# The drain of an attention stage reordered on five engines, and TensorE's flag branch with the token mixers in both arms

## The chip, the cores and the metric

One Trainium2 chip, one of its cores. The metric is the device time in microseconds (us) of one execution of the program. The kernel before takes 621.71 us, the median of 3 runs (621.22 to 622.42).

## The reference

Three layers in float32, one after the other. The input is 4 batches, 8 heads, 768 tokens, 48 features a head.

```python
# 1: gated linear attention, per head, token by token
state = f[t][:, None] * state + outer(k[t], v[t])      # f = sigmoid(f_logit)
y[t]  = q[t] @ state
# 2: token mixer on x = y with the heads side by side (768 x 384 per batch)
theta = x @ w_theta
mix   = w_tok_r @ (x * cos(theta)) + w_tok_i @ (x * sin(theta))
u     = x + mix
x2    = u + relu(u @ w_ch)
# 3: gated net
h = relu(x2 @ w_in);  u, v = halves of h;  v = layernorm(v)
out = (u * (w_spatial @ v + b_spatial)) @ w_out
```

## The kernel before, in words

**Attention** works on 16 pairs of heads, in a software pipeline. `pipeline(eng, stages)` gives each engine a list of (step, lag). In round n, a step with lag L handles pair n - L. Within a round an engine keeps strictly to its list. Rounds 16 to 19 (20 on SyncE) are the drain: no new pair begins and the last one, pair 15, runs out. Its PSUM banks are four `att_ps` (scores), `kt_ps`, `kv_ps` and two `y_ps`. A pair's result leaves as `y_out` (ScalarE, y_ps to y_sb) and `store` (SyncE, y_sb to the DRAM tensor xT). `y_out` of pair p waits until the store of pair p - 2 has landed.

All matmuls of the later layers are split: a float32 operand becomes a high and a low part (`split_hi` on ScalarE, line 73; `split_lo` on VectorE, line 78), and `three` (line 1054) issues hi x hi, hi x lo and lo x hi.

**The token mixer** handles a batch in six blocks s of 128 tokens. For each block: `turn(s)` on TensorE (three transposes into small_ps) and `xn_out(s)` on ScalarE; `theta(s)` on TensorE (9 matmuls into theta_bank); `to_turns(s)` on ScalarE; `reduce(s)` on VectorE (four operations); `trigs(s)` on ScalarE (abs, sin, cos); `multiply(s)` on VectorE; `z_up(s)` on ScalarE and `z_down(s)` on VectorE split the product z. Then `mix(s, third)` on TensorE: three thirds of 12 matmuls each into the six mix_ps banks. For the first batch each block also needs its part of the mixing weights: a load, `weights_up(s)` on ScalarE, `weights_down(s)` on VectorE. TensorE's list is mix(0,0), theta(2), mix(0,1), turn(3), mix(0,2), mix(1,0), theta(3), mix(1,1), turn(4), and so on. theta_bank and small_ps share PSUM with att_ps 0 and 1, mix_ps 0 to 5 with att_ps 2 and 3, kt_ps, kv_ps, y_ps 0 and 1.

The work on block 0 of the first batch is laid into attention's drain. SyncE's `load_first` (round 16, behind `load_rest` of pair 15 and ahead of the store of pair 11) loads w_theta (576 KB), both halves of x (576 KB each) and the weights of blocks 0 and 1 (768 KB each). ScalarE: `theta_hi` (round 17, last but y_out), `first_x` (round 18: x_hi and the Sin table load), `first_angles` (round 19, ahead of y_out of pair 15: weights_up(0), xn_out(0), to_turns(0), trigs(0)), `first_z` behind the pipeline. TensorE: `first_theta` (turn(0), theta(0); round 19, ahead of `attended` of pair 15), then turn(1) and theta(1) behind the pipeline. VectorE: `theta_lo` and `first_x` in round 18, weights_down(0) to z_down(0) behind the pipeline.

**The flag.** The fast attention is valid only for bounded decays. `row_tops` and `turn_tops` find the largest sum, VectorE writes `flag`, and each engine runs a branch of its own on it: with the flag set, the engines redo attention in another form (`attention_any_decay`). Here the flag is 0 and every engine jumps over that body. The mixers' code stands behind it. The remaining weights (blocks 2 to 5 and w_ch) are loaded by SyncE's `rest`, once the last store has landed (`load_weights`, line 1263).

## Time and profile before

| | |
|---|---|
| median of 3 runs | 621.71 us |
| the profiled execution | 619.17 us |
| its span, first to last instruction | 617.2 us |
| mean granted TensorE clock | 0.989 |
| TensorE matmuls busy (PE) | 580.9 us, 94% |
| VectorE (DVE) busy | 367.0 us, 59% |
| ScalarE (ACT) busy | 290.6 us, 47% |
| GpSimd (POOL) busy | 34.7 us, 6% |
| TensorE idle behind "issue" ahead of mix_ps | 2.0 us |
| TensorE idle behind "issue" ahead of gate_ps | 4.1 us |

Attention takes the first 121 us or so, the token mixer runs to about 363 us, the gated net to the end. In the page of 40 slices (15.4 us each) TensorE's digits are 9 but for the first slice (0), the last (8), and the seventh to ninth, from about 93 to 139 us: 8, 7, 8. That is the end of attention and the start of the token mixer. A share of busy time is an average over stages; what a change of the drain is worth is read from the drain's own rows.

### The profile page before, as it was taken

What the parts mean: (1) busy time and instruction counts of PE and PEld (TensorE: products, weight loads), DVE (VectorE), ACT (ScalarE), POOL (GpSimd) and SP (SyncE); (2) the same over time, 40 slices, a digit from 0 to 9 for tenths busy, and PEclk for the clock granted to TensorE, in tenths of its full rate; (3) what the DMA queues carried; (4) which work ended last, traced back from release to release, by engine and by line L of the source; (5) the groups of instructions that cost most, each with busy time, mean ns of one, the idle gap of its engine ahead of it and who ended that gap; (6) DMA issues with size and microseconds to landing.
All of it is one profiled execution on the core that took longest, in us unless ns stands there. A gap on an engine that the chain in (4) does not pass through costs nothing.

```text
span 617.2 us, 11905 instructions
## 1 busy us (share of the span) xinstructions
PE 580.9 (94%) x4226; PEld 559.9 (91%) x4226; DVE 367.0 (59%) x614; ACT 290.6 (47%) x509; POOL 34.7 (6%) x66
## 2 busy tenths in 40 slices
PE   0999998789999999999999999899999999999998
PEld 0888887689999999999999998898999899989997
DVE  7899998466776538454955557557145713571151
ACT  5799996765553335242644225415331533153112
POOL 3232332000000000000000000000000000000000
PEclk9999999879999999999999999899999999999999
DMA  7879999262410231022013243500040001000102
GB/s 187 201 228 246 267 252 314 59 219 93 192 38 27 65 102 39 25 76 89 0 43 115 76 144 109 207 2 1 25 129 2 0 25 51 0 1 27 52 0 78
DMA packets 31546, 58.76 MB, mean 95 GB/s; under 512 B 3728, under 2 KB 23184, under 8 KB 31504
## 3 DMA queue, kind: packets, MB, share of 16 engines
q1 hardware_dynamic: 31504, 58.21, 31.4%
q8 instruction: 25, 0.41, 0.3%
q14 instruction: 17, 0.14, 0.1%
HBM read 44.04 MB, written 14.16 MB: 94 GB/s over the span
## 4 chain that ended last, share of the span: by engine, by line
PE 72%; DVE 3%; issue 3%; ACT 1%; DMA 1%; DVEq 0%; ACTq 0%; SPq 0%
PE mix_ps L1054 24%; PE gate_ps L1054 16%; PE ringc L1054 10%; PE theta_bank L1054 10%; PE small_ps L1054 10%; PE small_ps L1436 1%; DVE stats L1998 1%; DVE w_lo L78 1%; DMA wc_stage<-in_wC_dram 1%; ACT w_hi L73 0%; ACT v L1848 0%; DVE vn L2016 0%; DVE ang L1574 0%; DVE ang L1571 0%; DVE z L1590 0%
## 5 line engine op out<-in xcount | busy, mean ns | idle before, releaser
L1054 PE MATMUL mix_ps<-w_lo,z_hi 128*128 128x384 f32 x288 | 97.3, 338 | 2.0 <-issue 2.0
L1054 PE MATMUL mix_ps<-w_hi,z_hi 128*128 128x384 f32 x288 | 99.0, 344 | 0.0
L1054 PE MATMUL mix_ps<-w_hi,z_lo 128*128 128x384 f32 x288 | 97.6, 339 | 0.0
L1054 PE MATMUL gate_ps<-w_hi 128*128 128x384 f32 x192 | 64.9, 338 | 4.1 <-issue 4.1
L1054 PE MATMUL gate_ps<-w_hi,w_lo 128*128 128x384 f32 x192 | 64.7, 337 | 0.0
L1054 PE MATMUL gate_ps<-w_lo,w_hi 128*128 128x384 f32 x192 | 64.7, 337 | 0.0
L1054 PEld LDWEIGHTS mix_ps<-w_hi,z_lo 128*128 128x128 f32 x288 | 54.6, 190 | 2.2 <-issue 2.2
L1054 PEld LDWEIGHTS mix_ps<-w_lo,z_hi 128*128 128x128 f32 x288 | 54.6, 190 | 0.0
L1054 PEld LDWEIGHTS mix_ps<-w_hi,z_hi 128*128 128x128 f32 x288 | 54.6, 189 | 0.0
L73 ACT ACTIVATE g_hi<-gate 128x384 fp32r<-128x384 f32 x32 | 16.8, 526 | 78.6 <-DVE gate L2048 78.6
L2044 DVE TENSOR_TENSOR gate<-gate_ps,b_all 128x384 f32<-128x384 f32 x32 | 17.8, 557 | 59.7 <-PE gate_ps L1054 59.5
L78 DVE TENSOR_TENSOR xt_lo<-xt,xt_hi 128x1152 fp32r<-128x1152 f32 x16 | 21.4, 1352 | 45.8 <-ACT xt_hi L73 45.8
L1054 PEld LDWEIGHTS gate_ps<-w_hi 128*128 128x128 f32 x192 | 36.6, 191 | 4.3 <-issue 4.3
L1590 DVE TENSOR_TENSOR z<-z,xn 128x384 f32<-128x384 f32 x48 | 24.6, 555 | 26.0 <-ACT z L1321 26.0
L1304 ACT ACTIVATE turns<-theta_bank 128x384 f32<-128x384 f32 x24 | 11.8, 490 | 53.4 <-PE theta_bank L1054 53.4
L1054 PEld LDWEIGHTS gate_ps<-w_lo,w_hi 128*128 128x128 f32 x192 | 36.5, 190 | 0.0
L1054 PEld LDWEIGHTS gate_ps<-w_hi,w_lo 128*128 128x128 f32 x192 | 36.5, 190 | 0.0
L1315 ACT ACTIVATE turns<-ang 128x384 f32<-128x384 f32 x24 | 12.6, 526 | 49.2 <-DVE ang L1578 49.2
L411 PE MATMUL kt_ps<-heads_first,ks 112*128 112x112 f32 x80 | 12.1, 286 | 20.1 <-DVE ks L560 20.0
L468 PE MATMUL y_ps<-att,v_raw 128*48 128x128 f32 x384 | 26.4, 291 | 3.5 <-ACT y_sb L378 3.5
L411 PEld LDWEIGHTS kt_ps<-heads_first,ks 112*128 112x128 f32 x80 | 8.5, 150 | 23.1 <-issue 17.2
L309 POOL TENSOR_SCALAR_AFFINE_SELECT att<-att 128x384 f32<-128x384 f32 x32 | 27.2, 872 | 33.9 <-ACT att L371 33.9
(163 smaller groups left out, 1417.1 us busy)
## 6 DMA issues: line engine op xcount, KB each, us to landing
f_raw<-in_fT_dram SPq DMA_DIRECT2D x32, 144.0 KB, 3.9
k_raw<-in_kT_dram SPq DMA_DIRECT2D x32, 144.0 KB, 3.3
q_raw<-in_qT_dram SPq DMA_DIRECT2D x32, 144.0 KB, 3.8
v_raw<-in_vC_dram SPq DMA_DIRECT2D x16, 288.0 KB, 4.0
xT<-y_sb SPq DMA_DIRECT2D x32, 144.0 KB, 3.7
xt<-xT SPq DMA_DIRECT2D x8, 576.0 KB, 4.0
w_raw<-in_wB_dram SPq DMA_DIRECT2D x6, 768.0 KB, 6.7
u<-xT SPq DMA_DIRECT2D x8, 576.0 KB, 5.0
```

The costliest lines, as they stand in the source:

```text
L73: return act.activation(hi, x, ACT.Copy)
L78: return dve.tensor_tensor(lo, x, hi.bitcast(F32), ALU.subtract)
L309: pool.affine_select(out=group, in_=group, compare_op=ALU.is_ge, fill=0.0, base=0, pattern=[[0, 3], [1, CHUNK]], channel_multiplier=-1).th ...
L411: last = pe.transpose(kt_ps_[:, c * PAIR:c * PAIR + ROWS], ks[b % 2][:, c * CHUNK:(c + 1) * CHUNK], heads_first[:, :])
L468: pe.matmul(y_ps_[half][rows, cols], values(b, hd, c), att[i][:, n * CHUNK:(n + 1) * CHUNK], start=(c % 3 == 0), stop=False)
L1054: done = pe.matmul(out, a, b, start=(first and n == 0), stop=(last and n == len(terms) - 1))
L1304: act.activation(turns[s % 2][:, :], theta_bank[:, 0:DMODEL], ACT.Copy, bias=MAGIC, scale=TURN_INV).then_inc(turns_done.h, 1)
L1315: act.activation(turns[i][:, :], ang[i][:, :], ACT.Abs).then_inc(mag_done.h, 1)
L1436: last = pe.transpose(small_ps[:, k * 128:(k + 1) * 128], xt[:, k * SEQ + s * 128:k * SEQ + (s + 1) * 128], ident[:, :])
L1590: dve.tensor_tensor(z[i][:, cols], z[i][:, cols], part(xn, s * DMODEL, DMODEL), ALU.mult)\
L1998: dve.bn_stats(stats[i][:, :], v[i][:, :]).then_inc(stats_done.h, 1)
L2044: dve.tensor_tensor(cols, gate_ps[g % 4][:, 0:HALF], part(b_all, th * HALF, HALF), ALU.add)\
```

## The change

It changes the order of steps in the drain, where two waits of TensorE stand, and how TensorE's code is laid out. The arithmetic is the same.

SyncE: w_theta is loaded in round 16 ahead of pair 15's own loads; each store now stands ahead of the mixer's loads of its round; x's first half goes in round 16, the weights of block 0 and x's second half in round 17, the weights of block 1 in round 18.

```diff
-            pipeline(sp, [(load_f, 0), (load_rest, 1), (load_first, 1), (store, 5)], 5, 2 * UNROLL)
+            pipeline(sp, [(load_f, 0), (load_theta, 1), (load_rest, 1), (store, 5), (load_first, 1), (load_mixing(0), 2), (load_mixing(1), 3)],
+                     5, 2 * UNROLL)
...
-            def load_early():
-                load(0)(FIRST)
-                load(1)(FIRST)
-                for n in range(2):
-                    sp.dma_start(w_raw[:, weights(n)], wB[:, weights(n)]).then_inc(wb_late[n], 16)
+            def load_first_x():
+                load(0)(FIRST)
+            def load_first_mixing(n):
+                sp.dma_start(w_raw[:, weights(n)], wB[:, weights(n)]).then_inc(wb_late[n], 16)
+                if n == 0:
+                    load(1)(FIRST)
```

ScalarE, TensorE and VectorE, the lists of the pipeline:

```diff
-            pipeline(act, [(neg_logs, 1), (keys_out, 3), (decays, 2), (growths, 2), (scores_copy, 3), (chunk_ends, 2), (theta_hi, 2),
-                           (first_x, 3), (first_angles, 4), (y_out(0), 4), (y_out(1), 4)])
-            m["first_z"]()
+            pipeline(act, [(neg_logs, 1), (keys_out, 3), (theta_hi, 2), (decays, 2), (growths, 2), (scores_copy, 3), (chunk_ends, 2),
+                           (first_turns, 3), (first_z, 4), (y_out(0), 4), (y_out(1), 4), (first_x, 2)])
...
-            pipeline(pe, [(turn, 3), (scores(0), 3), (scores(1), 3), (first_theta, 4), (attended(0), 4), (attended(1), 4), (states, 3),
-                          (carried(0), 4), (carried(1), 4), (turn_tops, 3)])
+            pipeline(pe, [(turn, 3), (scores(0), 3), (scores(1), 3), (attended(0), 4), (attended(1), 4), (turn_tops, 3), (first_theta, 3),
+                          (states, 3), (carried(0), 4), (carried(1), 4)])
...
-            pipeline(dve, [(sums, 2), (scores_out(0), 3), (scores_out(1), 3), (theta_lo, 3), (keep_in_range, 0), (scale_queries, 2),
-                           (scale_keys, 2), (state_sums, 3), (row_tops, 2), (first_x, 3)])
+            pipeline(dve, [(sums, 2), (scores_out(0), 3), (scores_out(1), 3), (first_x, 3), (top_to_flag, 3), (first_angles, 3),
+                           (keep_in_range, 0), (scale_queries, 2), (scale_keys, 2), (state_sums, 3), (row_tops, 2), (theta_lo, 2)])
```

On ScalarE `first_x` is now x_hi(0) alone; `first_turns` is the Sin table load, weights_up(0), xn_out(0), to_turns(0); `first_z` is trigs(0), z_up(0). On VectorE `top_to_flag` is the wait for TensorE's turned tops and the two operations that make the flag (before: behind the pipeline); `first_angles` is weights_down(0), reduce(0); `first_z`, behind the pipeline, is multiply(0), z_down(0).

TensorE's mix: the wait for the low part of z moves from ahead of the block to ahead of the first group's lo x hi products, and both of these products come last in each group. The wait for the y_ps banks moves from ahead of turn(2) to ahead of mix(0,2).

```diff
                     if third == 0:
                         pe.wait_ge(zhi_done.h, zhi_done.at(b, s + 1))
-                        pe.wait_ge(zlo_done.h, zlo_done.at(b, s + 1))
...
+                        for r in range(2):
+                            z = part(z_hi[i], r * DMODEL + d * 128, 128)
+                            pe.matmul(out, z, w_hi[:, weights_of[r]], start=(s == 0 and r == 0), stop=False)
+                            pe.matmul(out, z, w_lo[:, weights_of[r]], start=False, stop=False)
+                        if g == 0:
+                            pe.wait_ge(zlo_done.h, zlo_done.at(b, s + 1))
+                        for r in range(2):
+                            last = pe.matmul(out, part(z_lo[i], r * DMODEL + d * 128, 128), w_hi[:, weights_of[r]],
+                                             start=False, stop=(s == ST - 1 and r == 1))
...
+                def y_banks(b):
+                    if first(b):
+                        for at in y_out:
+                            pe.wait_ge(*at)
                 batches(pe, [
-                    (mix(0, 0), 1), (theta(2), 1), (mix(0, 1), 1), (turn(3), 1), (mix(0, 2), 1),
+                    (mix(0, 0), 1), (theta(2), 1), (mix(0, 1), 1), (turn(3), 1), (y_banks, 1), (mix(0, 2), 1),
```

TensorE's branch: before, `If(flag > 0)` holds the other attention alone and both mixers stand behind it. After, the mixers stand in the arm for flag 0, which comes first, and once more behind the other attention.

```diff
+        @block.tensor
+        def _(pe):
+            def mixers():
+                mixer["tensor"](pe)["rest"]([attended["a_out"]], [attended["y_sbd"]])
+                gated_tensor(pe)
+
+            pe.wait_ge(flag_ready, 1)
+            with pe.If(pe.value_load(flag[0:1, 0:1], min_val=0, max_val=1) < 1):
+                mixers()
+            with pe.Else():
+                any_decay_tensor(pe)
+                mixers()
```

## Rows read from the trace of the kernel before

**Rows 1.** Busy by stretch: the stretch's length; PE, PEld, DVE, ACT, POOL; clock, DMA.

```profile
125.00:130.00 5.00, 3.61 (x12) 3.61 (x12) 2.95 (x6) 3.64 (x6) 0.00 (x0) 0.54 0.66 209
```

**Rows 2.** Timeline, TensorE: start, duration, engine, line, tiles, [idle before <- its releaser].

```profile
101.75 1.34 PE L478 MATMUL y_ps<-qs,state 48*48 48x128 f32 x20
...
108.88 2.80 PE L468 MATMUL y_ps<-att,v_raw 128*48 128x128 f32 x24 [3.48 <-ACT y_sb L378]
...
123.64 0.52 PE L1436 MATMUL small_ps<-ident,xt 128*128 128x128 f32 x3 [2.71 <-ACT xn L1295]
123.93 0.41 PE L1054 MATMUL mix_ps<-w_hi,z_hi 128*128 128x384 f32 x1
126.39 0.48 PE L1054 MATMUL mix_ps<-w_lo,z_hi 128*128 128x384 f32 x1 [2.04 <-issue]
...
145.16 0.34 PE L1054 MATMUL mix_ps<-w_hi,z_hi 128*128 128x384 f32 x1
```

**Rows 3.** The chain that ended last, in order of time: start, length, what.

```profile
126.39 3.68 PE mix_ps L1054 x11
130.06 2.62 PE theta_bank L1054 x9
...
147.40 1.56 PE theta_bank L1054 x9
```

**Rows 4.** Timeline, ScalarE, same columns as rows 2.

```profile
100.34 0.84 ACT L339 ACTIVATE w_dn<-csum 112x768 f32<-112x768 f32 x1 [1.28 <-DVE csum L534]
...
103.08 1.17 ACT L73 ACTIVATE w_hi<-w_raw 128x1152 fp32r<-128x1152 f32 x1
108.24 0.87 ACT L378 ACTIVATE y_sb<-y_ps 112x384 f32<-112x384 f32 x2 [3.99 <-DMA xT<-y_sb]
...
111.40 1.28 ACT L1372 ACT_TABLE_LOAD   x1
...
113.98 1.48 ACT L73 ACTIVATE w_hi<-w_raw 128x1536 fp32r<-128x1536 f32 x1
...
119.23 0.52 ACT L1315 ACTIVATE turns<-ang 128x384 f32<-128x384 f32 x1 [2.54 <-DVE ang L1578]
...
123.00 0.49 ACT L1295 ACTIVATE xn<-small_ps 128x384 f32<-128x384 f32 x1 [0.31 <-issue]
```

**Rows 5.** Timeline, VectorE, same columns.

```profile
105.77 1.35 DVE L78 TENSOR_TENSOR w_lo<-w_raw,w_hi 128x1152 fp32r<-128x1152 f32 x1
...
115.49 1.76 DVE L78 TENSOR_TENSOR w_lo<-w_raw,w_hi 128x1536 fp32r<-128x1536 f32 x1 [0.88 <-ACT w_hi L73]
117.16 0.35 DVE L1565 TENSOR_SCALAR turns<-turns 128x384 f32<-128x384 f32 x1
...
120.78 1.03 DVE L1590 TENSOR_TENSOR z<-z,xn 128x384 f32<-128x384 f32 x2 [1.58 <-ACT z L1321]
122.72 0.96 DVE L78 TENSOR_TENSOR z_lo<-z,z_hi 128x768 fp32r<-128x768 f32 x1 [0.91 <-ACT z_hi L73]
...
133.25 0.36 DVE L1565 TENSOR_SCALAR turns<-turns 128x384 f32<-128x384 f32 x1
...
140.22 0.95 DVE L78 TENSOR_TENSOR z_lo<-z,z_hi 128x768 fp32r<-128x768 f32 x1
```

**Rows 6.** Timeline, SyncE's DMA issues: start, time over which they were issued, line.

```profile
92.20 0.80 SPq L238 DMA_DIRECT2D k_raw<-in_kT_dram  x2
...
97.72 24.52 SPq L265 DMA_DIRECT2D xT<-y_sb  x10
```

**Rows 7.** Timeline of all engines from 119 us, SyncE's issues.

```profile
121.46 0.78 SPq L265 DMA_DIRECT2D xT<-y_sb  x2
...
125.82 1.07 SPq L1263 DMA_DIRECT2D w_raw<-in_wB_dram  x2
```

**Rows 8.** The tile w_raw, its loads of 576 and 768 KB.

```profile
DMA to landing us min/median/max: 4.5/6.2/10.3
```

**Rows 9.** DMA by queue, 124.0 to 124.5 us: packets, MB, share of 16 engines.

```profile
q8 instruction: 1, 0.02, 11.6%
```

More of the change, by code:

```diff
@@ L252, in load_rest, with load_theta, load_mixing, f @@
                              vC[p.times(1), :, :, :].rearrange("h p x -> p h x")).then_inc(v_in[b].h, 16)
+            def load_theta(p, b):
+                if last_pair(p):
+                    sp.dma_start(w_raw[:, W_THETA:W_MIX], wB[:, W_THETA:W_MIX]).then_inc(w_in, 16)
             def load_first(p, b):
                 if last_pair(p):
-                    sp.dma_start(w_raw[:, W_THETA:W_MIX], wB[:, W_THETA:W_MIX]).then_inc(w_in, 16)
                     for c in x_out:
                         sp.wait_ge(c.h, 32 * 3)
-                    m["first"]()
+                    m["first_x"]()
+            def load_mixing(n):
+                def f(p, b):
+                    if last_pair(p):
+                        m["first_mixing"](n)
+                return f
             def store(p, b):
@@ L1039, in _ @@
                 mixer["vector"](dve)["redo"]()
+        return tensor
 def half_of_tokens(t, th, at=0):
@@ L1270, in rest @@
                 sp.wait_ge(mix_done.h, mix_done.at(Step(None, 1, BATCH - 1), GROUPS))
-            return {"open": opened, "first": load_early, "redo": redo, "rest": rest}
+            return {"open": opened, "first_x": load_first_x, "first_mixing": load_first_mixing, "redo": redo, "rest": rest}
         def pool(eng):
@@ L1467, in f @@
                             pe.wait_ge(u_done.h, u_done.at(b.back(1), g + 1))
-                        last = three(pe, mix_ps[g][:, 0:HALF],
-                                     [(both(z_hi[i], z_lo[i], r * DMODEL + d * 128, 128),
-                                       both(w_hi, w_lo, W_MIX + (2 * s + r) * SEQ + th * HALF, HALF))
-                                      for r in range(2)], first=(s == 0), last=(s == ST - 1))
+                        out = mix_ps[g][:, 0:HALF]
+                        at = [W_MIX + (2 * s + r) * SEQ + th * HALF for r in range(2)]
+                        weights_of = [slice(at[r], at[r] + HALF) for r in range(2)]
+                        for r in range(2):
+                            z = part(z_hi[i], r * DMODEL + d * 128, 128)
+                            pe.matmul(out, z, w_hi[:, weights_of[r]], start=(s == 0 and r == 0), stop=False)
+                            pe.matmul(out, z, w_lo[:, weights_of[r]], start=False, stop=False)
+                        if g == 0:
+                            pe.wait_ge(zlo_done.h, zlo_done.at(b, s + 1))
+                        for r in range(2):
+                            last = pe.matmul(out, part(z_lo[i], r * DMODEL + d * 128, 128), w_hi[:, weights_of[r]],
+                                             start=False, stop=(s == ST - 1 and r == 1))
                         if s == ST - 1:
@@ L1530, in redo, with rest @@
                 pe.wait_ge(redone, REDO_ALL)
-            def rest(banks_free):
-                for at in banks_free:
+            def rest(scores_out, y_out):
+                for at in scores_out:
                     pe.wait_ge(*at)
                 turn(2)(FIRST)
+                def y_banks(b):
+                    if first(b):
+                        for at in y_out:
+                            pe.wait_ge(*at)
                 batches(pe, [
-                    (mix(0, 0), 1), (theta(2), 1), (mix(0, 1), 1), (turn(3), 1), (mix(0, 2), 1),
+                    (mix(0, 0), 1), (theta(2), 1), (mix(0, 1), 1), (turn(3), 1), (y_banks, 1), (mix(0, 2), 1),
                     (mix(1, 0), 1), (theta(3), 1), (first_values(0), 2), (first_values(1), 2), (channel(0), 2), (mix(1, 1), 1), (turn(4), 1), (mix(1, 2), 1), (channel(1), 2),
@@ L1907, in _, with tensor @@
                 (y_out, 2), (x_hi, 0), (w_up(5), 1), (gate_up, 1)], 2)
-        @block.tensor
-        def _(pe):
+        def tensor(pe):
             for c in (u_ps, vs_ps, y_ps):
@@ L2129, in attention_and_mixers @@
                              main, tail_hi, tail_lo, qT, kT, fT, vC, xT)
-        attention_any_decay(nc, sems, block, mixer, attended, waits_passed, flag, flag_ready, qT, kT, fT, vC, xT)
+        any_decay_tensor = attention_any_decay(nc, sems, block, mixer, attended, waits_passed, flag, flag_ready, qT, kT, fT, vC, xT)
         @block.sync
@@ L2141, in _ @@
             mixer["scalar"](act)["rest"]([attended["x_out0"], attended["x_out1"]])
-        @block.tensor
-        def _(pe):
-            mixer["tensor"](pe)["rest"]([attended["a_out"], attended["y_sbd"]])
         @block.vector
@@ L2153, in attention_and_mixers @@
                 banks.enter_context(nc.psum_tensor(f"mixer_bank{_}", [128, 512], F32))
-            gated_net(nc, sems, block, gates, mixer, waits_passed, w_hi, w_lo, in_hi, in_lo, xt, xt_hi, xt_lo, eps, early, late, stage,
+            gated_tensor = gated_net(nc, sems, block, gates, mixer, waits_passed, w_hi, w_lo, in_hi, in_lo, xt, xt_hi, xt_lo, eps, early, late, stage,
                       wC, bias, x2T, out)
+        @block.tensor
[9 more added lines that the diff above has]
+                mixers()
 _INS = ["qT", "kT", "fT", "vC", "wB", "wC", "bias"]
```

178 lines of the change are left out of this document (92 added, 86 removed).

## The prediction

> **What bounds the kernel now.** I read the page of slices first, then the timelines of the stretch in which its TensorE digits dip, then the chain of waits. Outside that stretch TensorE issues matmuls back to back almost everywhere, so the end moves only if TensorE's steady work begins earlier. Inside it, TensorE loses time in four places. It stands 3.48 us from 105.40, waiting for a y_sb copy [rows 2]; ScalarE had itself waited 3.99 us for a store to land [rows 4], and that store was issued at 97.72, behind five loads of the mixer [rows 6]. It stands 2.71 us ahead of turn(2), waiting for xn_out(1) [rows 2]. One matmul into mix(0,0) it stands 2.04 us more behind "issue", a wait for nothing that semaphores show [rows 2], just when one block of instructions is fetched [rows 9]. And then it runs at the low level of its clock: the granted clock is 0.54 from 125 to 130 us, which is the 1.2 GHz level for nearly all of it, after those two stops [rows 1]. The reader should see that 20 matmuls take 6.30 us there, where nine take 1.56 later, 0.173 each [rows 3].
>
> **The change, step by step.** I walk the drain with durations from the rows; semaphore hops are inside the gaps between rows.
>
> *Loads.* w_theta moves ahead of pair 15's loads, so it is issued by 92.2 [rows 6]. With the median landing of 6.2 us it is there at 98.4, with the longest, 10.3, at 102.5 [rows 8]. theta_hi (1.17) then fits into ScalarE's 1.28 us of idle time ahead of 100.34 [rows 4] and costs nothing; in the bad case it costs its 1.17 as before. Pair 15's k, q and v queue behind 576 KB more. At 209 GB/s [rows 1] that is 2.8 us; k and q are used about 9 us after issue, so it is hidden. The store of pair 11 moves ahead of all mixer loads but w_theta: issued some 2.5 us earlier and behind 2.7 MB less, it lands well ahead of 103. That removes the 3.99 and with it the 3.48. What is late next is y_ps itself: carried(13) ends at 101.75 + 1.34 = 103.09 [rows 2], just as ScalarE gets there (103.08, where theta_hi stood [rows 4]). The weights of block 0 go one round later, behind the store of pair 12, which stands right behind the 97.72 in time [rows 6]: I estimate 99.4. They land between 103.9 and 109.7 [rows 8]; I take the median, 105.6.
>
> *ScalarE.* y_out(13), keys_out, scores_copy and x_hi(0) took from 108.24 to 111.40, 3.16 us [rows 4]. The same four now start at 103.1 and end at 106.3. The table load (1.28) brings 107.6, weights_up(0) (1.48) 109.0, xn_out(0) and to_turns(0) (0.49 each) 110.0. These last stand ahead of y_out(14), which TensorE needs for pair 15; carried(14) is done only at 111, so they hide there.
>
> *TensorE, round 18.* From 105.4: attended(14) at full clock, about half of 2.80 [rows 2], then the flag's matmul and turn(0); x_lo(0) on VectorE, behind x_hi(0) at 105.1 and its own scores, ends near 107.5 (1.35 [rows 5]); theta(0), nine matmuls, ends at 109.1. states(15) and carried(14) end at 111.0.
>
> *VectorE.* The flag's two small operations cost under 0.5 us and their wait is met by 107. weights_down(0) 109.0 to 110.8 (1.76), reduce(0) to 112.8 (2.07, from 117.16 [rows 5] to 119.23 [rows 4]). Behind it is queued state_sums(15), for which attended(1) of pair 15 waits: a new wait of about 1.7 us on TensorE, from 111.8 to 113.5. Then pair 15 ends at 115.6, turn(1) and theta(1) at 117.6. Were state_sums ahead of the angles, this would be gone; but the chain of angles ends later anyway, so it costs little.
>
> *The chain that sets mix(0,0).* reduce(0) 112.8, trigs(0) 114.35 (1.55, from 119.23 [rows 4] to 120.78 [rows 5]), multiply(0) 115.4, z_up(0) 116.3, y_out(15) 117.1, ScalarE's own branch 0.31, xn_out(1) 0.49: 117.9 [rows 4]; turn(2) and the hop, 123.49 to 123.93 before, 0.44. mix(0,0) begins at 118.25 where it began at 123.93 [rows 2]. **First term: 5.7 us.**
>
> *The branch.* TensorE then jumped over the other attention's code; now the code it needs follows the branch. The 2.04 goes if the jump caused it, stays if it was something else. I take it as gone: a fetch of instructions fell into this very stop [rows 9], and no other engine's state explains it (zhi and zlo were ready at 122.7 and 123.7 [rows 5]). The bounds are 0 and 2.04. **Second term: 2.0 us.** GpSimd's and SyncE's branches are as they were. In exchange TensorE jumps over the second arm at its very end. Such a stop, 2.04 us after the last matmul, lies beside the last output copy and store, so it costs nothing; were it twice as long it would cost about 1.5.
>
> The Trainium skill speaks to this edit, in "Runtime: NRT & Kernel Launch", section on instruction fetch mechanics: fetch is purely sequential, and a taken branch whose target is outside the resident window forces a fetch before work goes on. By it the stop ahead of mix goes. That one engine's stop differs from ScalarE's 0.31 for the same branch [rows 4] it does not explain. No other term here uses it.
>
> *The clock.* With the stops of 2.71 and 2.04 gone TensorE works from 113.5 on with gaps under 0.5 us, so it should stay at 2.4 GHz. Twenty matmuls in 6.30 become 3.5 [rows 3]. **Third term: 2.8 us**, bounds 0 and 2.8. The new wait of 1.7 us is shorter than the 3.48 before; the low level may still be granted at some place in 105 to 118, but there the ScalarE and VectorE chain has the say.
>
> *Reordered products.* Six matmuls per group before and after, each with its weight load: 0. The later wait for z_lo gives blocks four matmuls, 0.7 us, of slack. The later wait for y_ps banks (0 to about 0.5 us) is contained in the first term.
>
> *Given back.* Before, z_lo(2) was ready at 141.17 [rows 5] and mix(2,0) began at 145.16 [rows 2]: 4.0 us of slack. The three terms move TensorE 10.5 us and z only by 5.7 or so. So the slack is used up. By hand: multiply(1) 123.0, x_lo(1) (1.35), weights_down(1) (1.76) to 126.5, z_lo(1) to 127.4; TensorE wants mix(1,0) at 126.4 and its lo products at 127.1. It waits some 0.3. Then VectorE's round (133.25 to 141.17, 7.9 us [rows 5]) is shorter than TensorE's: 36 mix matmuls, nine of theta and a turn, 8.1. In the round with the next batch's x_lo (1.3 more) it falls short again by 0.2. The weights of blocks 2 on are issued 4.4 us behind the last store, as before (121.46 to 125.82 [rows 7]), about 121.5, and the first is wanted at 131: hidden. **Fourth term: -0.5 us.**
>
> Sum: 5.7 + 2.0 + 2.8 - 0.5 = 10.0 us. The profiled execution of 619.17 us (span 617.2 and 2.0 around it) becomes 609.2. The median of the runs is 2.5 above it, so 621.7 becomes 611.7. What comes after the first batch moves as a whole, the 4.1 us stop ahead of gate_ps included, which hangs on loads that TensorE's progress releases.
>
> **The rivals.**
>
> *A. The stop at the first mix stays, and with it the low clock.* For it: "issue" names no cause, and a block boundary can fall there in any layout. Against it: the fetch at that moment [rows 9]. Then terms two and three go, z has more time and term four shrinks to 0: gain 5.7, 616.0 us.
>
> *B. The chain of ScalarE and VectorE arrives 2 us later than I walk it*, because x's half, w_theta or a hop is late, or the end jump is exposed. No slack is left to absorb it, so each us counts fully: gain 8, 613.7 us. For it: my walk allows hardly any hop. Against it: it is anchored on stretches that contain the hops.
>
> *C. Slower.* weights_up(0) now stands on ScalarE ahead of xn_out(0), to_turns(0) and y_out(14), and reduce(0) on VectorE ahead of state_sums(15). So one late load, the weights of block 0, holds the whole of pair 15, its store, and the load of all later weights. The place has 2 us of slack (105.6 against 107.6) and from there each us is paid in full. It decides against the change once the load lands behind 117.6, 18 us after issue; at 20 us the gain is -2 and the time 623.7. For it: the DMA engines are loaded at this point, and four requests are ahead. Against it: 10.3 us is the longest such load seen [rows 8].
>
> *D. The end is set by something fixed to time*, such as weights of the gated net, and the drain only moves idle time: 621.7. Against it: those loads wait for buffers that the mixer frees.
>
> **How the numbers follow.** Forecast 0.52, B 0.20, A 0.16, D 0.05, C 0.07. Faster by over 0.2% (1.2 us, about what this measurement can tell): the first three, 0.88. Within 0.2%: D, 0.05. Slower: 0.07. The range reaches from 609.6 (term four zero, and the new 1.7 us wait of round 19 not on the path) to 616.7 (A with 0.7 us of B's lateness).
>
> **What would show it.** Right: no y_sb copy waits for a store; theta_hi begins before 100; mix(0,0) begins at 118 to 119; no "issue" ahead of mix; the granted clock from 120 to 130 is 1; mix(2,0) begins near 135, with z_lo(2) less than 1 us before or behind. Wrong: an "issue" of 2 us at the first mix (A); table load or weights_up waiting for a DMA (B, C); TensorE idle ahead of mix blocks 1 to 4 for longer than 0.5 us in all; a span that ends over 2.5 us behind the last matmul plus its copy.

## The result, and the profile after

The changed kernel takes **612.17 us** (median of 4 runs, 611.62 to 613.41) where the kernel before, run beside it, takes 621.47 (620.64 to 622.42): a ratio of **0.9853, with a 95% interval of 0.9832 to 0.9874**. The forecast was 611.7. The profiled execution took 611.62 us with a span of 609.7; before it was 619.17 with 617.2. So the profiles lie 7.5 us apart and the medians 9.3, and much of what follows is about that difference and about which part of the change earned it.

The page of the kernel after: busy time per engine, then the slices for TensorE and its clock (each digit a fortieth of the span, in tenths).

```profile
span 609.7 us, 11888 instructions
...
PE 577.4 (95%) x4226; PEld 555.4 (91%) x4226; DVE 365.9 (60%) x614; ACT 289.9 (48%) x509; POOL 35.6 (6%) x66
...
PE   0899999899998999999999997999999999999997
...
PEclk9899999999999999999999998999999999999999
```

TensorE has the same 4226 matmuls. Of the dip of three slices from 93 to 139 us (8, 7, 8) one 8 is left, in the eighth slice (107 to 122 us). The same stretch as [rows 1] now:

```profile
125.00:130.00 5.00, 4.91 (x27) 4.69 (x28) 3.22 (x8) 2.11 (x5) 0.00 (x0) 1.00 0.88 263
```

The granted clock is 1.00, that is 2.4 GHz, where it was 0.54. TensorE's timeline after, which answers to [rows 2] (start, duration, tiles, and in brackets the idle time before and its releaser):

```profile
112.18 0.86 PE L481 MATMUL y_ps<-att,v_raw 128*48 128x128 f32 x12 [1.58 <-issue]
...
116.51 0.42 PE L1492 MATMUL mix_ps<-w_hi,z_hi 128*128 128x384 f32 x1
116.77 0.34 PE L1493 MATMUL mix_ps<-w_lo,z_hi 128*128 128x384 f32 x1
...
120.24 0.34 PE L1492 MATMUL mix_ps<-w_hi,z_hi 128*128 128x384 f32 x1
...
125.09 0.45 PE L1492 MATMUL mix_ps<-w_hi,z_hi 128*128 128x384 f32 x1 [0.20 <-DVE w_lo L78]
...
133.51 0.34 PE L1492 MATMUL mix_ps<-w_hi,z_hi 128*128 128x384 f32 x1
...
167.21 0.44 PE L1492 MATMUL mix_ps<-w_hi,z_hi 128*128 128x384 f32 x1 [0.83 <-DVE u L1648]
...
184.70 0.52 PE L1456 MATMUL small_ps<-ident,xt 128*128 128x128 f32 x3 [1.78 <-DVE x L1690]
```

Of the three stops of [rows 2] none is left: the second matmul of mix(0,0) follows the first by 0.26 us. One new stop of 1.58 us stands ahead of attended(1), the second half of pair 15, and two waits on VectorE have come up later, at 167.21 and 184.70. At the second of these the kernel before waits too, but 0.67 us:

```profile
132.53 0.34 PE L1054 MATMUL mix_ps<-w_hi,z_hi 128*128 128x384 f32 x1
...
193.96 0.52 PE L1436 MATMUL small_ps<-ident,xt 128*128 128x128 f32 x3 [0.67 <-DVE x L1658]
```

ScalarE's timeline after, which answers to [rows 4], and SyncE's issues, which answer to [rows 6]:

```profile
97.47 1.15 ACT L73 ACTIVATE w_hi<-w_raw 128x1152 fp32r<-128x1152 f32 x1
...
101.61 0.86 ACT L388 ACTIVATE y_sb<-y_ps 112x384 f32<-112x384 f32 x2
...
104.89 1.28 ACT L1394 ACT_TABLE_LOAD   x1
106.19 1.49 ACT L73 ACTIVATE w_hi<-w_raw 128x1536 fp32r<-128x1536 f32 x1
...
115.60 0.49 ACT L1315 ACTIVATE xn<-small_ps 128x384 f32<-128x384 f32 x1
```

```profile
88.48 0.38 SPq L256 DMA_DIRECT2D w_raw<-in_wB_dram  x1
...
92.97 1.62 SPq L274 DMA_DIRECT2D xT<-y_sb  x2
...
97.87 0.51 SPq L1270 DMA_DIRECT2D w_raw<-in_wB_dram  x1
```

theta_hi (97.47) sits in ScalarE's gap, y_out(13) (101.61) waits for no store, and neither the table load nor weights_up(0) (106.19) waits for its load, although the weights of block 0 were issued 8.3 us before.

**Where the time went.** Executions differ in how far attention has got by the same point. As a mark I take the copy w_dn with which ScalarE enters the steady rounds (31.27 before, 30.08 after) and count from there; "lead" is how much earlier than before the kernel after is.

| place | before, from the mark | after, from the mark | lead |
|---|---|---|---|
| mix(0,0) | 92.66 | 86.43 | 6.23 |
| mix(0,1) | 101.26 | 90.16 | 11.10 |
| mix(2,0) | 113.89 | 103.43 | 10.46 |
| the wait for x, 193.96 and 184.70 | 162.69 | 154.62 | 8.07 |
| first gate_ps | 357.29 | 349.09 | 8.20 |
| end of ScalarE's last output copy | 583.58 | 576.20 | 7.38 |
| end of the span | 585.93 | 579.62 | 6.31 |

The last line and the 1.19 us by which the mark itself lies earlier make the 7.5 us between the two spans. TensorE gains 11.1 us by mix(0,1) and gives nearly half of it back: 3.0 until batch 1, 0.7 more later, 1.1 behind the last copy.

### The profile page after: what moved, and what is told of

Read it like the earlier page. It is cut to its first block, busy times and chain, and to the rows that moved or that the text cites. A ratio compares the mean times of both kernels' runs of the same rounds, so it can differ in the third digit from the quotient of the medians.

```text
span 609.7 us, 11888 instructions
## 1 busy us (share of the span) xinstructions
PE 577.4 (95%) x4226; PEld 555.4 (91%) x4226; DVE 365.9 (60%) x614; ACT 289.9 (48%) x509; POOL 35.6 (6%) x66
## 4 chain that ended last, share of the span: by engine, by line
PE 65%; DVE 4%; issue 2%; ACT 1%; DMA 1%; DVEq 0%; ACTq 0%; SPq 0%
PE gate_ps L1073 17%; PE ringc L1073 11%; PE small_ps L1073 10%; PE theta_bank L1073 9%; PE mix_ps L1492 6%; PE mix_ps L1497 6%; PE mix_ps L1493 6%; PE mix_ps L1073 2%; PE small_ps L1456 1%; DVE stats L2031 1%; DVE w_lo L78 1%; DMA wc_stage<-in_wC_dram 1%; ACT w_hi L73 0%; DVE z_lo L78 0%; ACT v L1882 0%
## 5 line engine op out<-in xcount | busy, mean ns | idle before, releaser
L1497 PE MATMUL mix_ps<-w_hi,z_lo 128*128 128x384 f32 x288 | 73.6, 337 | 0.0
L1497 PEld LDWEIGHTS mix_ps<-w_hi,z_lo 128*128 128x128 f32 x288 | 51.8, 188 | 0.4 <-DVE z_lo L78 0.4
L73 ACT ACTIVATE z_hi<-z 128x768 fp32r<-128x768 f32 x24 | 20.2, 841 | 17.8 <-PE mix_ps L1497 9.7
```

What stands on the lines that cost most here:

```text
L73: return act.activation(hi, x, ACT.Copy)
L1497: last = pe.matmul(out, part(z_lo[i], r * DMODEL + d * 128, 128), w_hi[:, weights_of[r]], start=False, stop=(s == ST - 1 and r == 1))
```

## The experiments

All are edits of the kernel before or of the kernel after. Times are medians; the number of timed runs stands with each. The runs of the kernel before on the same chip were 621.43 (first group), 621.74 (second) and 621.09 (third).

**Before again: is the profile of before typical?** The unchanged kernel (first group, one run).

> The kernel before, unchanged, for a second profile. In the first pair of profiles VectorE of the kernel after runs 1.48 us ahead already in attention's steady rounds (60 to 100 us), where the change does nothing. Theory, that this is scatter of the start: this profile's first masked scores, keys and decays lie anywhere within 1.5 us of the first profile's, the idle times of TensorE in the drain (3.48, 2.71, 2.04 us) return within 0.2 us. Rival, that the changed code does it: the steady rounds lie where they lay (w_dn of the pair at 60.14 us within 0.3 us).

It took 621.16 us, with a span of 619.2 and the mark at 30.45. TensorE's stop ahead of attended(14), then ScalarE's wait for the store:

```profile
109.91 2.80 PE L468 MATMUL y_ps<-att,v_raw 128*48 128x128 f32 x24 [5.63 <-ACT y_sb L378]
```

```profile
109.28 0.87 ACT L378 ACTIVATE y_sb<-y_ps 112x384 f32<-112x384 f32 x2 [6.15 <-DMA xT<-y_sb]
```

The store lands later than in the first profile: 6.15 us of wait and not 3.99. Here mix(0,0) starts 95.57 us behind the mark, 2.9 later. Of TensorE's three idle times (3.48, 2.71 and 2.04 us) the first is 5.63 here, the second 3.06 and the third 1.85, so my expectation that they return within 0.2 us missed for the first two. Most runs of before have a span near 619.6 and the granted clock of this one (0.98). I take this one for the usual execution and the profile that I predicted from for a quick one; only these two executions of before have a profile, and in the experiments below that keep the late store the wait is 4.12 us (branch alone) and 5.51 (stores behind loads). If so, that is why the medians are 9.3 apart and the profiles 7.5.

**After again: is the start part of the gain?** The changed kernel, unchanged (third group, 6 runs).

> The kernel after, unchanged, beside the next three on one chip. Its first profile had the earliest start of all (w_dn at 30.08 us, seven others 31.3 to 32.8), so its first four times may flatter it. Theory, the start is scatter: this profile starts anywhere from 30 to 33, span less start is 579.6 within 0.7 us; median 612 to 614 us. Rival, the early start belongs to the program: it is at 30.1 again.

614.19 us, ratio 0.9886 (0.9865 to 0.9907). The profile has the mark at 32.36, mix(0,0) 86.46 behind it and first gate_ps 349.20 behind it, the same as the first profile of after to 0.1 us. The span from the mark is 580.74, 1.1 more than 579.62 and outside the 0.7 that I had allowed: 0.7 of it lies behind the last copy and 0.4 ahead of it. So the mark's time is scatter, and a difference of a us between two such distances at the end is still scatter. Over the 14 profiles it is 30.1 to 32.8, with no order by kernel. The gain of the change is 7 to 9 us: 0.9886 here, 0.9853 in the first measurement.

**SyncE's order alone.** The kernel before with the new order of loads and stores and nothing else (second group, 4 runs).

```diff
...
-            pipeline(sp, [(load_f, 0), (load_rest, 1), (load_first, 1), (store, 5)], 5, 2 * UNROLL)
+            pipeline(sp, [(load_f, 0), (load_theta, 1), (load_rest, 1), (store, 5), (load_first, 1), (load_mixing(0), 2), (load_mixing(1), 3)], 5, 2 * UNROLL)
...
```

> The kernel before with SyncE's new order of loads and stores alone. Theory: the y_sb copy of pair 13 no longer waits for a store (4.0 to 6.2 us in two profiles of before), TensorE's stop of 3.5 to 5.6 us ahead of pair 14's attended goes with the low clock behind it, and the drain moves as a whole: 3.5 to 5.5 us faster than before (0.991 to 0.994). The rest of the gain of the full change needs the new lists. Rival, without the new lists the next wait (theta_hi, x_hi and the table load behind one another on ScalarE) takes its place: under 1.5 us.

614.74 us, 0.9884 (0.9867 to 0.99): 7.0 us faster, more than I expected. TensorE's timeline:

```profile
119.30 0.62 PE L1446 MATMUL small_ps<-ident,xt 128*128 128x128 f32 x3 [3.10 <-ACT xn L1305]
...
121.98 0.48 PE L1063 MATMUL mix_ps<-w_lo,z_hi 128*128 128x384 f32 x1 [1.70 <-issue]
```

```profile
120.00:125.00 5.00, 3.30 (x11) 3.12 (x11) 2.84 (x6) 2.95 (x6) 0.00 (x0) 0.50 0.47 147
```

The two later stops of before are still there, and the low clock behind them. What went is the stop for the store, and with it the low clock in attended(14), whose 24 matmuls took 2.80 us in [rows 2] and 1.52 here. In before again that was 5.63 us of stop and 1.28 of low clock, 6.9 together. My range of 3.5 to 5.5 us had the stops of the two profiles in it and left the clock out.

**Stores behind loads.** The kernel after with store 11 behind all mixer loads (first group, 12 runs).

```diff
-            pipeline(sp, [(load_f, 0), (load_theta, 1), (load_rest, 1), (store, 5), (load_first, 1), (load_mixing(0), 2), (load_mixing(1), 3)],
+            pipeline(sp, [(load_f, 0), (load_rest, 1), (load_theta, 1), (load_first, 1), (load_mixing(0), 1), (load_mixing(1), 1), (store, 5)],
```

> The kernel after with SyncE's order of before: in round 16 pair 15's loads, then w_theta, the halves of x and the weights of blocks 0 and 1, then the store of pair 11. Theory: the y_sb copy of pair 13 waits for that store again, some 4 us; theta_hi, now ahead of decays of pair 15, waits for w_theta a little too (0 to 1.5 us); the chain through x_hi(0), the angles and z is late by all of it: 4 to 6 us slower than the kernel after, 0.991 to 0.995 of before. Rival, the order of steps on the other engines alone brings the gain and the stores were hidden: within 1 us of the kernel after.

620.16 us, 0.9985 (0.9963 to 1.0006). The whole gain is gone: 6 us against after again, 8 against the first measurement of after, more than the 4 to 6 that I expected. ScalarE, then TensorE:

```profile
102.60 1.17 ACT L73 ACTIVATE w_hi<-w_raw 128x1152 fp32r<-128x1152 f32 x1 [0.71 <-DMA w_raw<-in_wB_dram]
...
112.01 0.87 ACT L388 ACTIVATE y_sb<-y_ps 112x384 f32<-112x384 f32 x2 [5.51 <-DMA xT<-y_sb]
```

```profile
112.64 2.80 PE L481 MATMUL y_ps<-att,v_raw 128*48 128x128 f32 x24 [3.93 <-ACT y_sb L388]
```

The low clock stands behind the stop again: these 24 matmuls take 2.80 us. With sync_only this settles the main cause from both sides: the order on SyncE's queue is worth 6 to 8 us, and the rest of the change gains nothing that these runs can tell when the store is late (0.9963 to 1.0006).

**The branch alone.** The kernel before with TensorE's mixers in both arms (first group, 12 runs).

```diff
...
+            def mixers():
...
+            with pe.If(pe.value_load(flag[0:1, 0:1], min_val=0, max_val=1) < 1):
+                mixers()
+            with pe.Else():
+                any_decay_tensor(pe)
+                mixers()
```

> The kernel before with TensorE's branch alone changed: the mixers in the arm for flag 0 and again behind the other attention. Theory: the 2.04 us issue stop at the first mix goes and with it the low clock of the next 20 matmuls (2.8), but VectorE's chain is not moved, and it was found to cap TensorE's lead at about 1.7 us at the start of batch 1; the jump at the end costs 1.1. So 0.5 to 1 us faster than before (ratio 0.998 to 1.000), with TensorE idle ahead of mix of batch 1 or of small_ps. Rival 1, the terms of the prediction add up freely: 4.8 us faster (0.992). Rival 2, the stop is not the jump's: it stays, 1 us slower (1.002).

621.32 us, 0.9996 (0.9978 to 1.0015): nothing. The stop in the first mix is gone, but:

```profile
125.51 0.87 PE L1435 MATMUL small_ps<-ident,xt 128*128 128x128 f32 x3 [3.08 <-ACT xn L1294]
...
193.91 0.52 PE L1435 MATMUL small_ps<-ident,xt 128*128 128x128 f32 x3 [1.77 <-DVE x L1657]
```

The wait for xn stays at 3.08 us, and of the stop saved 1.1 us come back at the wait for x in batch 1 (1.77 where 0.67 stood). First gate_ps is 0.4 us nearer the mark than in the first profile of before, 2.4 nearer than in before again; behind the last output copy the span lasts 4.03 us where it was 2.35. The low clock does not go with the stop either: from 125 to 130 us 0.66 is granted here, behind the wait of 3.08 us alone, and from mix(0,0) to mix(0,1) it takes 4.94 us, where it is 8.60 in before and 3.73 in after. So 1.2 us of low clock belong to the wait for xn, and the branch by itself cannot earn them.

**The branch undone.** The kernel after with the branch of before (first group, 6 runs).

```diff
-            with pe.If(pe.value_load(flag[0:1, 0:1], min_val=0, max_val=1) < 1):
-                mixers()
-            with pe.Else():
+            with pe.If(pe.value_load(flag[0:1, 0:1], min_val=0, max_val=1) > 0):
                 any_decay_tensor(pe)
-                mixers()
+            mixers()
```

> The kernel after with TensorE's branch as before (the other attention alone in it, the mixers once, behind it). Theory: the 2.0 us stop is back at the first mix, perhaps with a stretch at the low clock; TensorE had 3.0 us of lead over VectorE's chain at that point which it lost by 167 us, so only what exceeds 3.0 is paid (0 to 1.8 us), and the 1.1 us at the end comes back: within -1.1 and +0.8 us of the kernel after, that is 0.984 to 0.987 of before. Rival, all of it is paid: 4.8 us slower than the kernel after, 0.993 of before. Rival, the stop is not the jump's: no stop, and the time falls by the 1.1 us of the end.

615.57 us, 0.99 (0.9871 to 0.9929): 3.4 slower than the first measurement of after and 1.4 slower than after again, so my expectation (1.1 faster to 0.8 slower) missed. TensorE's timeline, the instruction fetches of 118 to 119 and of 121 to 122 us, and the clock:

```profile
121.13 0.52 PE L1456 MATMUL small_ps<-ident,xt 128*128 128x128 f32 x3 [1.80 <-issue]
121.40 0.42 PE L1492 MATMUL mix_ps<-w_hi,z_hi 128*128 128x384 f32 x1
...
123.95 0.67 PE L1492 MATMUL mix_ps<-w_hi,z_hi 128*128 128x384 f32 x1 [1.95 <-issue]
```

```profile
q8 instruction: 1, 0.02, 6.1%
...
q8 instruction: 1, 0.02, 5.8%
```

```profile
125.00:130.00 5.00, 5.00 (x24) 5.00 (x24) 4.22 (x4) 2.42 (x3) 0.00 (x0) 0.76 0.87 320
```

The jump costs **two** stops, each with one fetch: one at the target, 1.80 us, and one a few matmuls later, 1.95 us. The packets of each fetch lie just ahead of its stop (118.5 to 118.75 and 121.5 to 121.75 us), 2.2 to 2.6 us before TensorE goes on. In the kernel before there is a fetch at 120.0 to 120.25 us as well. By the same distance the stop that belongs to it would end by 122.9, and TensorE waits for xn until 123.64, which hid the first stop from me. 3.75 us of stops and the low clock cost 3.4 at first gate_ps (352.51 behind the mark, 349.09 in after). At the end the 1.1 us of the other jump are saved: the span ends 2.33 us behind the last copy.

This kernel is also the new lists with SyncE's new order and without the branch, so against sync_only (614.74, 0.9884 to this one's 0.99) it shows what the lists of ScalarE, VectorE and TensorE and the order of the products earn by themselves: nothing, first gate_ps even lies 0.7 us farther from the mark (352.51 against 351.82). They take away the wait for xn, and the jump's first stop, hidden until then, stands in its place. Lists and branch together bring first gate_ps 2.7 us nearer (349.09), of which the end jump takes 1.1 back.

**Arms swapped.** The kernel after, the arm with the other attention first (second group, one run).

```diff
-            with pe.If(pe.value_load(flag[0:1, 0:1], min_val=0, max_val=1) < 1):
+            with pe.If(pe.value_load(flag[0:1, 0:1], min_val=0, max_val=1) > 0):
+                any_decay_tensor(pe)
                 mixers()
             with pe.Else():
-                any_decay_tensor(pe)
                 mixers()
```

> The kernel after with the two arms in the other order: If(flag > 0): the other attention and the mixers; Else: the mixers. TensorE jumps over a longer stretch at the start and over nothing at the end. Theory: the two stops of the old branch return (about 1.8 ahead of turn(2), about 2.0 at the first mix), no longer than there although the jump is several times as far; the 1.1 us at the very end goes. Span within 1 us of old_branch once the start is taken off (582.2 us from the w_dn near 31 us to the end). Rival, a farther jump costs more: stops over 3 us each. Rival, the end is not the jump's: it stays at 3.4 us behind the last copy.

612.55 us. TensorE's timeline, and the instruction fetch of 121 to 122 us:

```profile
121.16 0.52 PE L1456 MATMUL small_ps<-ident,xt 128*128 128x128 f32 x3 [2.21 <-issue]
121.44 0.42 PE L1492 MATMUL mix_ps<-w_hi,z_hi 128*128 128x384 f32 x1
```

```profile
q8 instruction: 1, 0.02, 6.6%
```

I had expected the two stops of the old branch and a span of 582.2 us from the mark; there is one stop, and the span from the mark is 578.7. This jump goes over the other attention and one whole copy of the mixers, much farther, and has one stop of 2.21 us (1.80 in the last experiment, which jumps as far): distance is not what costs. The second fetch happens while TensorE works: behind the row of 121.44 the matmuls follow one another without a stop. So the second stop hangs on where in a fetched block the target lies, which I argue and did not vary on purpose. There is no jump at the end (2.35 us behind the last copy), and VectorE takes up most of the delay: mix(0,0) starts 89.53 us behind the mark, 3.1 later than in after, first gate_ps only 0.8 later. So the span from the mark is 0.9 us less than in after, a difference that one profile of each can't tell from scatter.

**Old order of the products.** The kernel after with z_lo wanted at the head of a mix block (third group, 6 runs).

```diff
+                        pe.wait_ge(zlo_done.h, zlo_done.at(b, s + 1))
...
-                        for r in range(2):
-                            z = part(z_hi[i], r * DMODEL + d * 128, 128)
...
+                        last = three(pe, mix_ps[g][:, 0:HALF],
```

> The kernel after with mix's products in the order of before and the wait for the low part of z ahead of the block. Theory: TensorE begins mix(1,0) 0.9 us later, but VectorE's chain takes that away again by the start of batch 1: within 0.5 us of the kernel after. Rival, TensorE pays it in every block in which z is just in time: 1 to 3 us slower.

613.45 us, 0.9877 (0.9856 to 0.9899), 0.7 less than after again, inside the intervals of both. TensorE now waits at mix(1,0):

```profile
128.00 0.42 PE L1073 MATMUL mix_ps<-w_hi,z_hi 128*128 128x384 f32 x1 [1.15 <-DVE z_lo L78]
```

but the 0.82 us wait on u later on is gone and first gate_ps is at the same place (349.10 behind the mark). A stop of TensorE that VectorE's chain needs anyway costs nothing: the reordered products bought nothing.

**One more VectorE operation.** The kernel after with one subtraction of the size of weights_down ahead of weights_down(3), which is in the first batch alone; its result is not used (second group, 4 runs).

```diff
...
                         dve.wait_ge(wb_hi, n + 2)
+                        if n == 3:
+                            dve.tensor_tensor(u_lo[:, 0:MIX_PART], w_hi[:, weights(n)].bitcast(F32), w_hi[:, weights(n)].bitcast(F32), ALU.subtract)
```

> The kernel after with one more VectorE operation of 128x1536 elements (1.7 us, its result unused) ahead of weights_down(3) in the first batch. Theory: from 113 to 167 us VectorE's chain of splits and angles sets the time, so all of it is paid: 1.5 to 1.9 us slower than the kernel after (0.9875 to 0.9885 of before). Rival, TensorE is the bound and VectorE has slack there: within 0.3 us of the kernel after.

615.59 us, 0.9903 (0.9886 to 0.9919), 1.4 slower than after again and 3.4 than the first measurement of after, which are of other groups. The distances say more. In this profile mix(0,0) already lies 0.7 us farther from the mark (87.17) than in after, ahead of the edit. From mix(0,0) to first gate_ps it takes 264.37 us, where it is 262.66 in after and 262.74 in after again: 1.6 to 1.7 more, the whole of the operation. Behind first gate_ps 0.9 to 1.2 us come back, and the two profiles of before differ by 0.9 there as well: the last copy ends 577.76 us behind the mark, 576.20 in after and 576.61 in after again. TensorE waits for w_lo at once, and 0.31 us more one block later:

```profile
145.09 0.44 PE L1492 MATMUL mix_ps<-w_hi,z_hi 128*128 128x384 f32 x1 [0.63 <-DVE w_lo L78]
```

So in this stretch of the kernel after VectorE's chain is the bound, or within half a us of it.

**Weights split in the gaps.** If VectorE is the bound there, its order matters. Its angles wait for ScalarE and ScalarE's sines wait for the angles; weights_up(s) and weights_down(s) need neither. This version moves them into those waits, for every block of the first batch (second group, 4 runs; third group, 5 runs).

```diff
...
-                    (z_up(1), 1), (to_turns(2), 1), (u_up(0), 2), (u_up(1), 2), (trigs(2), 1), (xn_out(3), 1), (weights_up(2), 1), (w_in_up(0), 1),
+                    (z_up(1), 1), (to_turns(2), 1), (u_up(0), 2), (u_up(1), 2), (weights_up(2), 1), (trigs(2), 1), (xn_out(3), 1), (w_in_up(0), 1),
...
-                    (z_down(1), 1), (reduce(2), 1), (u_down(0), 2), (u_down(1), 2), (multiply(2), 1), (weights_down(2), 1), (w_in_down(0), 1),
+                    (z_down(1), 1), (reduce(2), 1), (weights_down(2), 1), (u_down(0), 2), (u_down(1), 2), (multiply(2), 1), (w_in_down(0), 1),
```

> The kernel after with two more moves. Block 0: ScalarE makes xn and turns of block 0 ahead of the weights' high part, VectorE the angles ahead of the low part. Blocks 1 to 5 of the first batch: weights_up(s) stands behind to_turns(s) and weights_down(s) behind reduce(s), in the 1.6 us in which VectorE waits for the sines. Theory: block 0's chain is 1.0 us shorter, and VectorE's round falls from 7.9 to about 6.5 us, below TensorE's 8.1, so the 3.0 us of lead that TensorE lost by 167 us stay: 3 to 4.5 us faster than the kernel after, 607.7 to 609.2 us (0.978 to 0.981 of before), if the weights of block 2 land by 127 us. Rival, TensorE was the bound: 1 us or less. Rival, the weights' loads, wanted 3 us earlier, hold ScalarE: a wait for w_raw of 1 us or more takes their place.

> split_in_gap unchanged, to compare it with the kernel after on one chip. Theory: 3.0 to 4.0 us faster than the kernel after (3.8 by span less start). Rival: what its first runs showed was the start's scatter; under 2 us.

**609.60 us, 0.9804 (0.9788 to 0.982), and 610.11, 0.9835 (0.9811 to 0.9858)**: the fastest kernel here, 4.1 us below after again in the same group. VectorE, one round from turns to turns, and TensorE's wait for x:

```profile
124.99 0.35 DVE L1597 TENSOR_SCALAR turns<-turns 128x384 f32<-128x384 f32 x1
...
126.94 1.75 DVE L78 TENSOR_TENSOR w_lo<-w_raw,w_hi 128x1536 fp32r<-128x1536 f32 x1
128.60 1.03 DVE L1622 TENSOR_TENSOR z<-z,xn 128x384 f32<-128x384 f32 x2
...
131.42 0.35 DVE L1597 TENSOR_SCALAR turns<-turns 128x384 f32<-128x384 f32 x1
```

```profile
182.53 0.52 PE L1456 MATMUL small_ps<-ident,xt 128*128 128x128 f32 x3 [0.66 <-DVE x L1690]
```

The multiply that needs the sines follows right behind w_lo; the round is 6.4 us, less than TensorE's 8.1. The wait for u is gone, and the one for x is back at 0.66. First gate_ps lies 345.17 and 345.73 us behind the mark in the two profiles, 3.4 to 4.0 nearer than in after. Of that 0.4 to 1.0 is there at mix(0,0): with block 0's splits out of the way too, the new stop ahead of attended(1) is gone, and 0.57 us of waiting for y_sb is left. The rival that I had named shows in part: weights_up(2) on ScalarE now waits 1.78 and 1.37 us for its load, but no wait of TensorE follows from it.

**The same with arms swapped** (third group, 6 runs): both edits above.

> split_in_gap with the arms swapped as in arms_swapped, which showed one stop of 2.2 us ahead of turn(2), none at the mix, and the last 1.1 us back. Theory: with VectorE's round short nothing absorbs the 2.2 us at the start: 1 us slower than split_in_gap, 0.981 to 0.983 of before. Rival, the stop is absorbed as in arms_swapped: 1 us faster than split_in_gap, 0.978.

611.32 us, 0.9851 (0.982 to 0.9882). TensorE has one stop of 1.80 us ahead of turn(2), and the span ends 2.38 us behind the last copy where it was 3.48. From the mark the span is 576.2 against 575.7, and the median is 1.2 us higher, as expected, but both lie inside the scatter: unclear. It trades one jump for the other.

## Why the prediction was right

The time, 611.7, is 0.5 us from the measured 612.17. Its steps, one by one:

- **Loads and ScalarE: right.** With the mark 1.19 us earlier in the profile after, y_out(13) was due at 101.9 and came at 101.61; the table load was due at 105.1 and came at 104.89. weights_up(0) did not wait. Block 0's weights were issued at 97.87, where 98.2 was due.
- **The new wait behind reduce(0): right.** 1.58 us on TensorE, where 1.7 stood. The row says "issue" for it, but by the code attended(1) waits for state_sums(15), which VectorE does behind reduce(0), and that operation ends 0.1 us before TensorE goes on at 112.18:

```profile
111.33 0.75 DVE L591 TENSOR_TENSOR_SCAN state<-kv_ps,ends 112x288 f32<-112x288 f32 x1
```

- **First term, 5.7: right against the profile, low against before again.** 6.23 from the mark against the profile; against before again it is 9.1, where the store's wait is 2.2 us longer than in the profile that I had.
- **Second and third terms, 2.0 and 2.8: right for the change, not for their cause.** Between mix(0,0) and mix(0,1) the lead grows by 4.87, where 4.8 was forecast (by 3.75 against before again). The low clock is not the jump's alone, as the branch alone shows: the wait for xn had its part in it. And I held the stop in the mix for the whole price of the jump. It has two stops; the first was covered by the wait for xn. That it has a price of 3.75 us shows only where nothing covers it (old_branch).
- **The end jump: wrong, 0 against 1.1.** I had put one stop of 2.04 us there, beside the last output copy and store, "so it costs nothing". The span now ends 3.42 us behind the last copy (4.13 in after again, 4.03 in branch_only) where it ended 2.35 behind. ScalarE's last copy, and the instruction fetch of 606 to 607 us:

```profile
605.79 0.49 ACT L1923 ACTIVATE y<-ringc 128x384 f32<-128x384 f32 x1 [1.59 <-PE ringc L1073]
```

```profile
q8 instruction: 1, 0.02, 6.9%
```

No such fetch stands behind the last matmul in before, arms_swapped or gap_swapped, and all three have a tail of 2.35 to 2.38. Over all 14 profiles the tail is 2.33 to 2.38 us in the six without this jump and 3.35 to 4.13 in the eight with it. So the tail belongs to the jump. One stop of 2.04 us would have fitted into the 2.87 us that lie between the end of the last matmul and the end of the span in before; now they are 3.95. There is another fetch at 603.5 to 603.75 us, ahead of the last matmul's end, so I take it that this jump too has two stops; no row shows what TensorE does there. The case that I had named, a stop twice as long that costs about 1.5, is the one that came, and so did my sign of being wrong, an end over 2.5 us behind the last copy.

- **Fourth term, 0.5: this is the one that was mis-sized; it measures 3.0** from mix(0,1) to batch 1. I forecast 0.3 us at mix(1,0), 0.2 in the round with the next batch's x_lo, and otherwise set VectorE's round of 7.9 us against TensorE's 8.1, so that they would stay level. VectorE's timeline after:

```profile
132.79 0.95 DVE L78 TENSOR_TENSOR z_lo<-z,z_hi 128x768 fp32r<-128x768 f32 x1
...
157.36 0.95 DVE L78 TENSOR_TENSOR z_lo<-z,z_hi 128x768 fp32r<-128x768 f32 x1
...
163.78 0.96 DVE L78 TENSOR_TENSOR z_lo<-z,z_hi 128x768 fp32r<-128x768 f32 x1 [0.91 <-ACT z_hi L73]
164.66 0.35 DVE L1597 TENSOR_SCALAR turns<-turns 128x384 f32<-128x384 f32 x1
...
166.61 1.02 DVE L1648 TENSOR_TENSOR u<-mix_ps,u 128x384 f32<-128x384 f32 x2
...
173.61 0.95 DVE L78 TENSOR_TENSOR z_lo<-z,z_hi 128x768 fp32r<-128x768 f32 x1
```

Within batch 0 they do stay level: from 132.79 to 157.36 are three rounds, 8.19 us on the mean. What I did not count is the change of batch. There VectorE's list has the next angles (164.66) ahead of u (166.61), the next z_lo comes 9.83 us behind the last, and with its slack gone TensorE waits 0.83 us for u and then 1.78 us for x, where before waits 0.67.

The lead, taken block by block of TensorE's list, holds still but for four places, and these make up the 3.0. At mix(1,0) it falls by 0.64, from 11.10 to 10.46: the wait for w_lo listed with 0.20 us and one for z_lo too short to be listed, ahead of the row below. In the round with x_lo it falls by 0.18, as forecast. At the wait for u it falls by 1.09 and at the wait for x by 1.11. The listed times add up to less, since a listed wait leaves out what TensorE loses in starting again: the matmul of 125.09 and the next lie 0.29 us apart, where 0.17 is usual.

```profile
125.96 0.61 PE L1497 MATMUL mix_ps<-w_hi,z_lo 128*128 128x384 f32 x2
```

- **Rival A** (the stop stays) fell. **Rival B** had two halves: that the chain arrives late did not come, that the end jump is exposed did. **Rival C** (late weights of block 0) did not show: the loads of w_raw landed in 4.2, 6.0 and 6.7 us (least, median, most), where 10.3 was the most before. **Rival D** fell.

So that 611.7 met 612.17 to 0.5 us is luck. For the profiled execution I forecast 609.2 and it took 611.62, 2.4 more: 2.5 us too little for VectorE, 1.1 for the end and 0.7 for what is given back between, against a first term 0.5 too small and a mark 1.19 earlier. To that I added the 2.5 us by which the profile of before lay under its median; the profile of after lies only 0.55 under its own. The two errors cancel, and after again came to 614.19. The sign and the main cause stand by experiment: without the new order of stores and loads the rest of the change earns nothing (0.9985), and that order alone earns 7.0 us. The branch earns nothing by itself (0.9996) and 1.4 to 3.4 us once the lists have taken the wait for xn away, by which of the two measurements of after one takes, both of another group. The lists without the branch earn nothing. The prediction had these as terms that add up freely, which they are not.

The Trainium skill, "Runtime: NRT & Kernel Launch", section on instruction fetch mechanics, says that a taken branch to a target outside the resident blocks waits for a fetch. The runs agree, with a fetch at every such stop, and put a number to it: 1.8 to 2.2 us at the target.

## What to carry to other kernels

On one DMA queue put a store that frees a buffer ahead of every load whose use is further off: here that was 7 of the 7 to 9 us, from moving issues alone, and the other edits earned something only together. A saving on the bounding engine lasts only as far as the next engine's slack, so before adding up terms, count the busy time of that next engine over whole rounds, the fuller rounds too; then look for its work that depends on nothing and move it into its waits (4 us more here). Price a taken jump at both of its ends, see whether a wait hides a stop behind it before taking that wait away, and take the profile of before a second time if one wait on a DMA carries the sum.

## What the runs showed of the hardware that I had not expected

- A taken jump of TensorE costs one or two stops, each just behind one instruction fetch: 1.80 and 1.95 us (old_branch), 2.21 alone (arms_swapped, a far longer jump), 1.80 alone (gap_swapped, as long). As the last thing TensorE does it adds 1.0 to 1.8 us to the span.
- The same store, issued in the same place, held ScalarE 3.99 us in one execution of the kernel before and 6.15 in another; mix(0,0) came 2.9 us later in the second.
- The unchanged kernel after reaches the steady rounds at 30.1 us in one profile and at 32.4 in another (30.1 to 32.8 over all 14 profiles), so two spans say less than two distances from a common mark. At mix(0,0) and first gate_ps those agree to 0.1 us, at the end of the span they still differ by 1.1.
- Behind a long stop the low clock lasted into full work: in before again the granted clock is 0.79 from 105 to 110 us, a stretch in which TensorE is all but idle, and 0.52 from 110 to 115, when it is busy throughout. One stop of 1.58 us (after), of 1.80 (gap_swapped) or of 2.21 us (arms_swapped) cost no clock. Stops of 1.80 and 1.95 us with 0.9 us of work between them did (0.76 from 125 to 130 us, old_branch), and so did one wait of 3.08 us (0.66 in the same stretch, branch_only).
